# Reordered work at the first layer's beginning and at the layer change of a fused attention and two-layer expert kernel

## The chip, the cores and the metric

One core of a Trainium2 chip runs the whole program. The metric is device time in microseconds, lower is better. The engines are TensorE (PE, with its weight loads as PEld), VectorE (DVE), ScalarE (ACT), GpSimd (POOL) and SyncE (SP), which issues the DMAs.

## The reference

A decayed linear attention over 2 batches of 8 heads and 768 steps gives 1536 tokens of 512 features. They go through a gated layer of 1536 hidden features, and that through four experts of 1024.

```python
state = gamma * state + einsum('bhd,bhe->bhde', k[:, :, t], v[:, :, t])
y[:, :, t] = scale * einsum('bhd,bhde->bhe', q[:, :, t], state)
...
xn = x / rms * rms_g
h = silu(xn @ w_gate) * (xn @ w_val)
x = h @ w_out
...
for e in range(4):
    out += p[:, e:e + 1] * (maximum(x @ w1[e], 0) @ w2[e])
```

All in float32. `silu(g)` is `g / (1 + exp(-g))`, and `p` are the domain probabilities divided by their sum.

## The kernel before

**The arithmetic.** A float32 matmul is made of three: each operand is split into a high part (rounded, made by a copy) and a low part (operand minus high part), and `three` (L616) adds high by high, low by high and high by low in PSUM. On top of this every block product is a 2 by 2 block matrix product made with seven products instead of eight (M1 to M7, `PRODUCTS` for the up projections, `DOWNS` for the first layer's down projection). Its operands are the blocks A11, A12, A22 and four sums S1 to S4 of blocks for the tokens, and B11, B12, B21, B22 and T1 to T4 for the weights. Each of the seven operands of a side needs its own high and low part.

**The stages.** Twelve attention steps (`for n in range(NSTEP)` on each engine) fill `x_all`, and each three of them are normalised as they end. Then the tokens of the first layer come in two halves, `j` = 0 and 1 (the texts call their operand sets k = 0 and 1; k = 2 and 3 are the second layer's), and the hidden features in chunks `c` of 128. An up unit `q` is one chunk by one half: seven products of two k-tiles with three matmuls each, into three PSUM banks, 0 to 2 for even q and 3 to 5 for odd ones. The first units are (c, j) = (0,0), (1,0), (0,1), (1,1), (2,0), (3,0), (2,1), and so on: 24 units (`Q1`) in the first layer. Two units of one half form a pair `r`; its hidden blocks are summed and split too (`hidden_sum`, `hidden_hi`, `hidden_lo`, in four groups: A11; S2 and S3; A22 and A12; S1 and S4), and give 14 down steps (`down1`, L661), which alternate between banks 6 and 7. Step n waits for `posted` to reach n - 1, so a bank must have been taken out before it is written again. The pair's down steps are placed between the products of later units: pair 0's all in unit 3, two after each product (`LATE`), pair 1's in units 4 and 5 (`FIRST`, `SECOND`). The last pairs of the first layer and the second layer use `tile1` and `tile2` in place of the seven products. The second layer's units are 24 and on.

**Who does what.** ScalarE makes the high parts (`part_hi`, `hidden_hi`), copies products that are used twice out of PSUM (`copy_up`: M1, M6, M7 of each unit; M6, M7 and M4 wait for these copies, since they write the same bank), and applies silu. VectorE adds (`c11`, `c22_sum`, `c12`), multiplies (`hidden`), sums tokens and hidden blocks, makes low parts and takes the down steps out of PSUM (`post1`, `post3`, `post2`). GpSimd prepares all weights: four sums (`sum_w`), the high part in one instruction (`split_w_hi`), seven low parts (`split_w_lo`), and some low parts of the tokens, with S3 and once S4 as sums. M3 waits for `c22_ready`.

**What sets the order.** Each engine runs one queue in program order, written out by hand in the stretches that the change touches, with semaphores between engines. GpSimd's stands at L500 to L535: for k = 0 A22 then S3; then four of chunk 1's weights; for k = 1 A11, A12, sum S3, A22, S3, sum S4, S4; the low parts of the down weights (`split_wd_lo(0, 1)`, which first waits for VectorE's one); hidden groups 2 and 3 of pair 0; then the weights of chunk 2, 3, the down weights 1, chunk 4. SyncE's `load_w(c)` (L301) waits until chunk c - 1 has been split, as there is one raw buffer `w_raw` (places 0 to 3 the T sums, 4 to 7 the B blocks). `split_w_hi(c)` waits for the last product of the unit that last read the same of the two buffers. TensorE's order is that of `unit` (L705) with the calls from L726 on; M1 of units 1, 2 and 3 comes two products early, after M7 of the unit before, and the order is the same in both kernels.

## Time and profile before

| | |
|---|---|
| time, median of 3 runs | 842.86 us (842.85 to 845.74) |
| the profiled execution, time | 842.8 us |
| its span, first to last instruction | 841.0 us |
| TensorE busy | 824.5 us, 98% |
| VectorE, ScalarE, GpSimd busy | 549.2, 251.2, 467.7 us |
| TensorE clock granted | 0.999 of full |

Times in rows are microseconds from the span's start. A busy share is an average: this kernel has an attention stage until about 54, the first layer until about 340, overlapping with the second from there to the end. In a timeline, a group's length is from its first start to its last end, and the bracket tells how long the engine had been idle and what released it. Where an instruction waits for several semaphores, the one that came last by the profile is named.

### The profile page before, as it was taken

Reading aid. Unit: us, or ns where it says so; the run is one execution under the profiler, and the core shown is the slowest. Engines: PE = TensorE matmul, PEld = TensorE weight load, DVE = VectorE, ACT = ScalarE, POOL = GpSimd, SP = SyncE. Lnnn points to the kernel's source line nnn. Section 1 sums busy time; section 2 is a strip of 40 time slices with the busy share of each in tenths; the row PEclk is TensorE's granted clock in tenths of the full one; section 3 lists DMA queues with packets and bytes.
Section 4 is the critical chain, followed back from the end, with each engine's and each line's share of the span. In section 5 each row is a group of like instructions: output and inputs, shape, how many; then the busy total and the mean of one; then the engine's idle time right before and its main releaser. Section 6 shows DMA issues by size and latency. Waiting matters only on the chain.

```text
span 841.0 us, 13007 instructions
## 1 busy us (share of the span) xinstructions
PE 824.5 (98%) x4786; PEld 761.2 (91%) x4786; DVE 549.2 (65%) x878; ACT 251.2 (30%) x483; POOL 467.7 (56%) x506
## 2 busy tenths in 40 slices
PE   8998999999999999999999999999999999999998
PEld 8878889999999999789989889899898898898997
DVE  4798978888888868764545545545545545545545
ACT  3586223333333334322222222212212222222221
POOL 3899987968787849932736326326325425425100
PEclk9999999999999999999999999999999999999999
DMA  9801020001010010101100110110110110110003
GB/s 351 315 33 51 1 72 29 26 28 50 26 51 26 26 51 26 51 2 50 52 20 30 51 35 16 51 45 7 50 51 1 51 51 1 51 51 1 25 13 139
DMA packets 12877, 43.17 MB, mean 51 GB/s; under 512 B 1424, under 2 KB 1808, under 8 KB 12816
## 3 DMA queue, kind: packets, MB, share of 16 engines
q1 hardware_dynamic: 12528, 41.69, 14.0%
q8 instruction: 40, 0.66, 0.3%
q10 hardware_dynamic: 288, 0.65, 0.2%
q14 instruction: 21, 0.17, 0.1%
HBM read 39.19 MB, written 3.15 MB: 50 GB/s over the span
## 4 chain that ended last, share of the span: by engine, by line
PE 82%; POOL 9%; DVE 4%; DMA 2%; issue 2%; SPq 1%; ACT 0%; DVEq 0%; POOLq 0%
PE bank L620 27%; PE bank L618 27%; PE bank L619 27%; POOL x_lo L290 3%; POOL w_lo L399 2%; DMA ring<-qkv 2%; POOL w_raw L370 2%; POOL x_sum L286 1%; POOL wd_lo L440 1%; DVE x_sum L286 1%; POOL w_hi L392 1%; POOL h_lo L459 0%; DMA w_raw<-wu 0%; PE bank L547 0%; DVE x_lo L290 0%
## 5 line engine op out<-in xcount | busy, mean ns | idle before, releaser
L618 PE MATMUL bank<-x_hi,w_hi 128*128 128x384 f32 x784 | 264.2, 337 | 7.3 <-POOL w_lo L399 2.9
L620 PE MATMUL bank<-x_lo,w_hi 128*128 128x384 f32 x784 | 262.9, 335 | 0.0
L619 PE MATMUL bank<-x_hi,w_lo 128*128 128x384 f32 x784 | 262.8, 335 | 0.0
L1212 DVE SCALAR_TENSOR_TENSOR out_acc<-bank,p_norm,out_acc 128x512 f32<-128x512 f32 (+1 forms) x181 | 135.1, 747 | 127.2 <-PE bank L620 126.9
L618 PEld LDWEIGHTS bank<-x_hi,w_hi 128*128 128x128 f32 x784 | 147.2, 188 | 15.6 <-issue 6.7
L399 POOL TENSOR_TENSOR w_lo<-w_raw,w_hi 128x256 fp32r<-128x256 f32 x196 | 151.2, 806 | 3.0 <-ACT w_hi L761 0.8
L619 PEld LDWEIGHTS bank<-x_hi,w_lo 128*128 128x128 f32 x784 | 147.2, 188 | 5.5
L620 PE MATMUL bank<-wd_lo,h_hi 128*128 128x512 f32 (+1 forms) x386 | 152.0, 394 | 0.0
L619 PE MATMUL bank<-wd_hi,h_lo 128*128 128x512 f32 (+1 forms) x386 | 151.6, 393 | 0.0
L618 PE MATMUL bank<-wd_hi,h_hi 128*128 128x512 f32 (+1 forms) x386 | 150.0, 389 | 1.4 <-DVE out_acc L1208 1.2
L620 PEld LDWEIGHTS bank<-x_lo,w_hi 128*128 128x128 f32 x784 | 147.1, 188 | 0.0
L446 POOL TENSOR_SCALAR wd_hi<-wd_raw 128x1024 fp32r<-128x1024 f32 x17 | 18.6, 1096 | 209.2 <-DMA wd_raw<-wd 209.2
L794 ACT ACTIVATE u<-bank 128x384 f32<-128x384 f32 x112 | 55.1, 492 | 192.8 <-PE bank L620 192.7
L370 POOL TENSOR_TENSOR w_raw<-w_raw 128x256 f32<-128x256 f32 x112 | 91.2, 836 | 19.9 <-DMA w_raw<-wu 17.7
L820 ACT ACTIVATE h_hi<-bank 128x384 fp32r<-128x384 f32 x96 | 47.3, 492 | 137.9 <-PE bank L620 64.8
L620 PEld LDWEIGHTS bank<-wd_lo,h_hi 128*128 128x128 f32 x386 | 72.4, 188 | 15.2
L618 PEld LDWEIGHTS bank<-wd_hi,h_hi 128*128 128x128 f32 x386 | 72.5, 188 | 14.6 <-issue 2.8
L392 POOL TENSOR_SCALAR w_hi<-w_raw 128x1792 fp32r<-128x1792 f32 x26 | 46.3, 1780 | 69.6 <-PE bank L620 68.9
L619 PEld LDWEIGHTS bank<-wd_hi,h_lo 128*128 128x128 f32 x386 | 72.4, 188 | 11.9
L1158 DVE SCALAR_TENSOR_TENSOR h_lo<-bank,h_hi 128x384 fp32r<-128x384 f32 x96 | 53.2, 554 | 43.0 <-ACT h_hi L820 43.0
L1187 DVE TENSOR_TENSOR x_all<-bank,x_all 128x384 f32<-128x384 f32 x124 | 63.8, 549 | 2.8 <-PE bank L620 2.7
L794 ACT ACTIVATE m<-bank 128x384 f32<-128x384 f32 x56 | 27.5, 491 | 126.0 <-PE bank L620 126.0
(86 smaller groups left out, 994.2 us busy)
## 6 DMA issues: line engine op xcount, KB each, us to landing
w_raw<-wu SPq DMA_DIRECT2D x28, 512.0 KB, 4.4
ring<-qkv SPq DMA_DIRECT2D x23, 512.0 KB, 9.1
wd_raw<-wd SPq DMA_DIRECT2D x22, 512.0 KB, 3.6
out<-out_acc SPq DMA_DIRECT2D x11, 256.0 KB, 2.0
ring<-qkv ACTq DMA_DIRECT2D x1, 512.0 KB, 7.4
y_first<-t_y_decay SPq DMA_DIRECT2D x1, 256.0 KB, 8.0
out<-out_acc SPq DMA_DIRECT2D x2, 128.0 KB, 1.8
small_sb<-small ACTq DMA_DIRECT2D x1, 126.0 KB, 5.2
```

The costliest lines, as they stand in the source:

```text
L290: return engine.tensor_tensor(x_lo[j][:, XS[name], kt, :], operand(k, name)[:, kt, :], x_hi[j][:, XS[name], kt, :].bitcast(F32), ALU.subtract)
L370: return nc.gpsimd.tensor_tensor(w_raw[:, WS[to], :, :], w_raw[:, WS[a], :, :], w_raw[:, WS[b], :, :], ALU.subtract).then_inc(w_sums, 1)
L392: nc.gpsimd.tensor_scalar(w_hi[c % 2][:, :, :, :], w_raw[:, 0:7, :, :], 1.0, 1.0, ALU.mult, ALU.mult).then_inc(w_hi_ready, 1)
L399: nc.gpsimd.tensor_tensor(w_lo[c % 2][:, WS[ws], :, :], w_raw[:, WS[ws], :, :], w_hi[c % 2][:, WS[ws], :, :].bitcast(F32), ALU.subtract).t ...
L618: pe.matmul(dst, s_hi, m_hi, start=first, stop=False, skip_group_check=True)
L619: pe.matmul(dst, s_lo, m_hi, start=False, stop=False, skip_group_check=True)
L620: return pe.matmul(dst, s_hi, m_lo, start=False, stop=last, skip_group_check=True)
L794: nc.scalar.activation(tile[:, s, :], bank[3 * s][:, 0:TB], ACT.Copy).then_inc(u_copied, 1)
L820: nc.scalar.activation(h2_hi[q % 2][:, v, a, :], src, ACT.Relu).then_inc(hi_ready, 1)
L1158: nc.vector.scalar_tensor_tensor(out=h2_lo[q % 2][:, v, a, :], in0=src, scalar=0.0, in1=h2_hi[q % 2][:, v, a, :].bitcast(F32), op0=ALU.max ...
L1187: nc.vector.tensor_tensor(to, new, to, ALU.add).then_inc(posted, 1)
L1212: nc.vector.scalar_tensor_tensor(out=to, in0=new, scalar=p, in1=to, op0=ALU.mult, op1=ALU.add).then_inc(posted, 1)
```

## The change

- SyncE: the weights of chunk 3 are loaded into a buffer of their own, `w3_raw`, over memory that the squares used, after the last norm and after load 2 has landed. Load 4 then waits for chunk 2's split and load 3's landing, not for chunk 3's split.
- GpSimd: chunk 3's B blocks are read from `w3_raw`, and its high part takes two instructions. S3 comes before A22 for k = 0. `sum_4(1)`, `hidden_lo(0, 2)` and `hidden_lo(0, 3)` and, for k = 2, A22's low part go to VectorE.
- ScalarE: a new `post1` copies steps 0 to 7 of pairs 0 and 1 from banks 6 and 7 to `x_all`; the order of units 2 to 4 is written out; S2 before S3 for k = 1; at the layer change S3 of k = 2 before `hidden_hi3`, and M1 of unit 26 is copied before S4 of k = 3.
- VectorE: `post1` keeps only the additions for these pairs; two waits for down steps are added, in `hidden` and `hidden_sum`, which were implied by its posts before; the order from unit 1 to unit 3 and at the layer change is new.

```diff
@@ -147,6 +147,8 @@
...
+        w3_raw = at("w3_raw", [P, 4, 2, P], F32, LAST)
@@ -299,8 +301,15 @@
...
             def load_w(c):
+                if c == 3:
+                    sp.wait_ge(norm_done, 4)
+                    sp.wait_ge(w_in, 16 * c)
+                    sp.dma_start(w3_raw[:, :, :, :], wu[c]).then_inc(w_in, 16)
+                    return
                 if c >= 1:
-                    sp.wait_ge(w_ready, NP * c)
+                    sp.wait_ge(w_ready, NP * (c - 1 if c == 4 else c))
+                    if c == 4:
+                        sp.wait_ge(w_in, 16 * c)
                 sp.dma_start(w_raw[:, 4:8, :, :], wu[c]).then_inc(w_in, 16)
@@ -366,20 +375,27 @@
...
-            def w_op(to, a, b):
-                return nc.gpsimd.tensor_tensor(w_raw[:, WS[to], :, :], w_raw[:, WS[a], :, :], w_raw[:, WS[b], :, :],
-                                               ALU.subtract).then_inc(w_sums, 1)
+            def w_block(c, name):
...
+                if c == 3 and name[0] == "B":
+                    return w3_raw[:, WS[name] - 4, :, :]
+                return w_raw[:, WS[name], :, :]
...
+            def w_op(c, to, a, b):
+                return nc.gpsimd.tensor_tensor(w_block(c, to), w_block(c, a), w_block(c, b), ALU.subtract).then_inc(w_sums, 1)
...
                 pool.wait_ge(w_in, 16 * (c + 1))
-                w_op("T1", "B12", "B11")
-                w_op("T3", "B22", "B12")
+                if c == 3:
+                    pool.wait_ge(w_ready, NP * c)
+                w_op(c, "T1", "B12", "B11")
+                w_op(c, "T3", "B22", "B12")
...
                 pool.wait_ge(w_sums, 4 * c + 1)
-                w_op("T2", "B22", "T1")
+                w_op(c, "T2", "B22", "T1")
                 pool.wait_ge(w_sums, 4 * c + 3)
-                w_op("T4", "B21", "T2")
+                w_op(c, "T4", "B21", "T2")
@@ -389,14 +405,19 @@
...
                     pool.wait_ge(up_done, up_count(last_unit(c - 2), "M3"))
-                nc.gpsimd.tensor_scalar(w_hi[c % 2][:, :, :, :], w_raw[:, 0:7, :, :], 1.0, 1.0,
-                                        ALU.mult, ALU.mult).then_inc(w_hi_ready, 1)
+                if c == 3:
+                    nc.gpsimd.tensor_scalar(w_hi[c % 2][:, 0:4, :, :], w_raw[:, 0:4, :, :], 1.0, 1.0, ALU.mult, ALU.mult)
+                    nc.gpsimd.tensor_scalar(w_hi[c % 2][:, 4:7, :, :], w3_raw[:, 0:3, :, :], 1.0, 1.0,
+                                            ALU.mult, ALU.mult).then_inc(w_hi_ready, 1)
+                else:
+                    nc.gpsimd.tensor_scalar(w_hi[c % 2][:, :, :, :], w_raw[:, 0:7, :, :], 1.0, 1.0,
+                                            ALU.mult, ALU.mult).then_inc(w_hi_ready, 1)
...
                 for _, _, _, ws, _ in PRODUCTS[first:last]:
-                    nc.gpsimd.tensor_tensor(w_lo[c % 2][:, WS[ws], :, :], w_raw[:, WS[ws], :, :],
+                    nc.gpsimd.tensor_tensor(w_lo[c % 2][:, WS[ws], :, :], w_block(c, ws),
                                             w_hi[c % 2][:, WS[ws], :, :].bitcast(F32),
@@ -451,14 +472,6 @@
...
-            def hidden_lo(r, g):
...
-                pool.wait_ge(hid_hi_ready[g], r + 1)
-                pool.wait_ge(hid_sums, 4 * r + 4)
-                for i in range(GROUPS[g].start, GROUPS[g].stop):
-                    lo = nc.gpsimd.tensor_tensor(h1_lo[:, i, :], h1_raw[:, i, :], h1_hi[:, i, :].bitcast(F32), ALU.subtract)
-                lo.then_inc(hid_split[g], 1)
@@ -468,11 +481,6 @@
...
-            def sum_4(k):
-                pool.wait_ge(x_ready["S2"], k + 1)
-                token_sum(nc.gpsimd, k, "S4", slice(0, 1))
-                token_sum(nc.gpsimd, k, "S4", slice(1, 2)).then_inc(sum_ready["S4"], 1)
@@ -500,19 +508,16 @@
...
                     split_w_lo(1, 0, 3)
+            part_lo(0, "S3")
             part_lo(0, "A22")
-            part_lo(0, "S3")
             split_w_lo(1, 3, NP)
...
             part_lo(1, "S3")
-            sum_4(1)
             part_lo(1, "S4")
             split_wd_lo(0, 1)
-            hidden_lo(0, 2)
-            hidden_lo(0, 3)
             for p in range(1, D1):
@@ -525,7 +530,6 @@
...
             part_lo(2, "S3")
-            part_lo(2, "A22")
             split_w(F1 + 1)
@@ -811,6 +815,16 @@
...
+            def post1(r, first, last):
...
+                for i in range(first, last):
+                    n, s = first_part(r) + i, i % 2
+                    _, _, _, _, (half, a) = DOWNS[i // 2]
+                    act.wait_ge(down_done, n + 1)
+                    if r and i == 0:
+                        act.wait_ge(posted, n)
+                    nc.scalar.activation(x_all[r][:, 2 * half + s, a, :], bank[6 + s][:, 0:TB], ACT.Copy).then_inc(posted, 1)
@@ -857,7 +871,8 @@
...
                 s = q % 2
-                copy_up(q, "M1", m1)
+                if q > Q1 + 2:
+                    copy_up(q, "M1", m1)
                 copy_up(q, "M6", u2)
@@ -938,23 +953,45 @@
...
             part_hi(1, "S1")
+            part_hi(1, "S2")
             part_hi(1, "S3")
-            part_hi(1, "S2")
             copy_up(2, "M1", m1)
...
             part_hi(1, "S4")
+            copy_up(2, "M7", u3)
             hidden_hi(0, 0)
-            copy_up(2, "M7", u3)
             hidden_hi(0, 1)
             copy_up(3, "M1", m1)
+            hidden_hi(0, 2)
+            post1(0, 0, 2)
             silu(2, 0)
             silu(2, 1)
-            hidden_hi(0, 2)
             hidden_hi(0, 3)
-            unit1(3)
-            for q in range(4, QP):
+            post1(0, 2, 4)
+            copy_up(3, "M6", u2)
+            post1(0, 4, 6)
+            post1(0, 6, 8)
+            silu(3, 0)
+            copy_up(3, "M7", u3)
+            hidden_hi(1, 0)
+            silu(3, 1)
+            copy_up(4, "M1", m1)
+            hidden_hi(1, 1)
+            copy_up(4, "M6", u2)
+            hidden_hi(1, 2)
+            post1(1, 0, 2)
+            silu(4, 0)
+            copy_up(4, "M7", u3)
+            post1(1, 2, 4)
+            hidden_hi(1, 3)
+            silu(4, 1)
+            post1(1, 4, 6)
+            copy_up(5, "M1", m1)
+            post1(1, 6, 8)
+            unit1(5)
+            for q in range(6, QP):
                 unit1(q)
@@ -969,8 +1006,8 @@
...
             copy_up(Q1, "M1", m1)
+            part_hi(2, "S3")
             hidden_hi3(q, 1)
-            part_hi(2, "S3")
             hidden_hi3(q, 0)
@@ -1001,9 +1038,10 @@
...
             relu_hi(q, 0, 1, bank[3 * (q % 2)][:, 0:TB])
-            part_hi(3, "S4")
             act.wait_ge(c12_ready, q + 1)
             relu_hi(q, 1, 0, bank[3 * (q % 2) + 1][:, 0:TB])
+            copy_up(q + 1, "M1", m1)
+            part_hi(3, "S4")
             for q in range(Q1 + 2, NQ):
@@ -1105,6 +1143,8 @@
...
                     dve.wait_ge(c12_ready, q + 1)
+                    if v == 0 and 0 < q < QP:
+                        dve.wait_ge(down_done, first_part(q // 2 - 1) + 2)
                     x, y = bank[3 * s + 1][:, 0:TB], gate[:, s, :]
@@ -1116,6 +1156,8 @@
...
                 dve.wait_ge(hid_ready, 4 * r + blocks)
+                if to == "S3" and r:
+                    dve.wait_ge(down_done, first_part(r - 1) + 6)
                 if sums:
@@ -1176,15 +1218,12 @@
...
                     n, s = first_part(r) + i, i % 2
-                    name, _, _, _, (half, a) = DOWNS[i // 2]
+                    _, _, _, _, (half, a) = DOWNS[i // 2]
                     d = 2 * half + s
...
                     to, new = x_all[j][:, d, a, :], bank[6 + s][:, 0:TB]
-                    if r < J and name not in ("M2", "M5", "M3"):
-                        nc.vector.tensor_copy(to, new).then_inc(posted, 1)
-                    else:
-                        dve.wait_ge(posted, n - 1)
-                        nc.vector.tensor_tensor(to, new, to, ALU.add).then_inc(posted, 1)
+                    dve.wait_ge(posted, n if r < J and i == 8 else n - 1)
+                    nc.vector.tensor_tensor(to, new, to, ALU.add).then_inc(posted, 1)
@@ -1217,20 +1256,24 @@
...
                 c11(q)
-                post1(r, 0, 2)
+                if r >= J:
+                    post1(r, 0, 2)
                 hidden_sum(r, "S1")
                 c22_sum(q)
-                post1(r, 2, 4)
+                if r >= J:
+                    post1(r, 2, 4)
                 hidden_lo(r, 2)
                 hidden(q, 1)
-                post1(r, 4, 6)
+                if r >= J:
+                    post1(r, 4, 6)
                 c12(q)
...
                 r = q // 2 - 1
-                post1(r, 6, 8)
+                if r >= J:
+                    post1(r, 6, 8)
                 hidden_lo(r, 3)
@@ -1306,29 +1349,28 @@
...
             part_lo(1, "S1")
+            part_lo(1, "S2")
             c11(1)
-            part_lo(1, "S2")
+            sum_of(1, "S4")
             hidden(1, 1)
...
             hidden_sum(0, "S3")
+            c22_sum(2)
             split_wd_lo(0)
+            hidden_lo(0, 0)
+            hidden_sum(0, "S2")
             c11(2)
-            hidden_sum(0, "S2")
-            c22_sum(2)
-            hidden_lo(0, 0)
             hidden_sum(0, "S4")
+            hidden_lo(0, 1)
             hidden_sum(0, "S1")
-            hidden_lo(0, 1)
-            post1(0, 0, 2)
             hidden(2, 1)
             c12(2)
+            hidden_lo(0, 2)
             hidden(2, 0)
-            post1(0, 2, 4)
-            post1(0, 4, 6)
+            hidden_lo(0, 3)
             hidden_sum(1, "S3")
             c11(3)
-            post1(0, 6, 8)
             c22_sum(3)
@@ -1386,8 +1428,8 @@
...
             post3(RP, 6, 7)
+            c22_sum(q)
             part_lo(2, "S1")
-            c22_sum(q)
             post3(RP, 7, 8)
@@ -1401,8 +1443,9 @@
...
             post3(RP + 1, 0, 1)
+            part_lo(2, "A22")
+            part_lo(2, "S4")
             c22_sum(q)
-            part_lo(2, "S4")
             lo11(q)
@@ -1419,20 +1462,20 @@
...
             post2(q - 1, 0)
-            part_lo(3, "S1")
             post2(q - 1, 1)
             lo11(q)
+            c22_sum(q)
             sum_of(3, "S3")
-            c22_sum(q)
+            post2(q - 1, 2)
             lo22(q)
-            post2(q - 1, 2)
+            part_lo(3, "S1")
+            post2(q - 1, 3)
+            lo21(q)
             part_lo(3, "S2")
-            post2(q - 1, 3)
-            sum_of(3, "S4")
-            lo21(q)
             c12(q)
...
             post2(q - 1, 4)
+            sum_of(3, "S4")
             part_lo(3, "S3")
...
             part_lo(3, "S4")

```

## Rows read from the trace of the kernel before

**Rows 1.** The page: busy time by engine, and one costly group: busy, mean ns.

```profile
PE 824.5 (98%) x4786; PEld 761.2 (91%) x4786; DVE 549.2 (65%) x878; ACT 251.2 (30%) x483; POOL 467.7 (56%) x506
...
L794 ACT ACTIVATE u<-bank 128x384 f32<-128x384 f32 x112 | 55.1, 492 | 192.8 <-PE bank L620 192.7
```

**Rows 2.** Windows: stretch, its length, each engine's busy us (instructions), clock, DMA.

```profile
50.00:100.00 50.00, 44.91 (x276) 40.25 (x272) 45.44 (x65) 28.25 (x52) 48.80 (x46) 1.00 0.07 22
...
100.00:120.00 20.00, 17.92 (x101) 17.61 (x102) 16.23 (x27) 6.05 (x11) 16.17 (x20) 1.00 0.12 36
...
120.00:140.00 20.00, 20.00 (x118) 19.99 (x117) 17.12 (x31) 6.61 (x12) 16.91 (x19) 1.00 0.12 45
```

**Rows 3.** Timeline, TensorE 60 to 115, its stalls: start, length, line, [idle before <-releaser].

```profile
62.49 0.41 PE L618 MATMUL bank<-x_hi,w_hi 128*128 128x384 f32 x1 [0.51 <-POOL x_lo L290]
...
76.75 0.41 PE L618 MATMUL bank<-x_hi,w_hi 128*128 128x384 f32 x1 [1.35 <-DVE x_lo L290]
...
82.66 0.41 PE L618 MATMUL bank<-x_hi,w_hi 128*128 128x384 f32 x1 [1.51 <-issue]
...
88.30 0.41 PE L618 MATMUL bank<-h_hi,wd_hi 128*128 128x384 f32 x1 [0.96 <-POOL wd_lo L440]
...
100.05 0.41 PE L618 MATMUL bank<-h_hi,wd_hi 128*128 128x384 f32 x1 [0.58 <-DVE x_all L1187]
...
113.82 0.45 PE L618 MATMUL bank<-x_hi,w_hi 128*128 128x384 f32 x1 [2.02 <-POOL w_lo L399]
```

**Rows 4.** Timeline, GpSimd 58 to 108, instructions of one line merged (x count).

```profile
58.46 1.95 POOL L290 TENSOR_TENSOR x_lo<-x_all,x_hi 128x384 fp32r<-128x384 f32 x2
...
75.74 2.71 POOL L290 TENSOR_TENSOR x_lo<-x_sum,x_hi 128x384 fp32r<-128x384 f32 x2
...
78.42 2.48 POOL L286 TENSOR_TENSOR x_sum<-x_all,x_sum 128x384 f32<-128x384 f32 x2
...
83.78 5.88 POOL L440 TENSOR_TENSOR wd_lo<-wd_raw,wd_hi 128x256 fp32r<-128x256 f32 x6
...
89.62 3.93 POOL L459 TENSOR_TENSOR h_lo<-h_raw,h_hi 128x384 fp32r<-128x384 f32 x4
...
107.64 3.56 POOL L370 TENSOR_TENSOR w_raw<-w_raw 128x256 f32<-128x256 f32 x4 [3.58 <-DMA w_raw<-wu]
```

**Rows 5.** Timeline, VectorE 74 to 108, operations with both inputs in SBUF.

```profile
74.78 1.82 DVE L290 TENSOR_TENSOR x_lo<-x_sum,x_hi 128x768 fp32r<-128x768 f32 x1 [0.36 <-ACT x_hi L789]
...
83.14 1.10 DVE L1127 TENSOR_TENSOR h_lo<-h_raw,h_hi 128x384 fp32r<-128x384 f32 x1
...
86.19 1.49 DVE L1127 TENSOR_TENSOR h_lo<-h_raw,h_hi 128x768 fp32r<-128x768 f32 x1
...
107.21 0.55 DVE L1121 TENSOR_TENSOR h_raw<-h_a,h_raw 128x384 f32<-128x384 f32 x1
```

**Rows 6.** Timeline, ScalarE 80 to 83.

```profile
80.93 0.84 ACT L789 ACTIVATE x_hi<-x_sum 128x768 fp32r<-128x768 f32 x1 [2.37 <-POOL x_sum L286]
...
82.09 0.47 ACT L794 ACTIVATE u<-bank 128x384 f32<-128x384 f32 x1
```

**Rows 7.** Timeline, TensorE 320 to 360, its stalls at the layer change.

```profile
323.56 0.41 PE L618 MATMUL bank<-x_hi,w_hi 128*128 128x384 f32 x1 [0.31 <-DVE c L1085]
...
330.48 0.41 PE L618 MATMUL bank<-x_hi,w_hi 128*128 128x384 f32 x1 [0.41 <-POOL x_lo L290]
...
338.92 0.44 PE L618 MATMUL bank<-x_hi,w_hi 128*128 128x384 f32 x1 [0.92 <-POOL w_lo L399]
...
351.93 0.47 PE L618 MATMUL bank<-wd_hi,h_hi 128*128 128x512 f32 x1 [0.21 <-DVE out_acc L1208]
...
358.74 0.47 PE L618 MATMUL bank<-wd_hi,h_hi 128*128 128x512 f32 x1 [0.46 <-DVE out_acc L1208]
```

**Rows 8.** Timeline, GpSimd and VectorE 330 to 362.

```profile
330.30 1.97 POOL L290 TENSOR_TENSOR x_lo<-x_all,x_hi 128x384 fp32r<-128x384 f32 x2
...
361.44 0.74 DVE L1208 TENSOR_SCALAR out_acc<-bank,p_norm 128x512 f32<-128x512 f32 x1
```

## The prediction, made before the changed kernel ran

> **What bounds the kernel now.** I read the page's busy shares first: TensorE is busy 98% of the span, so only what it idles can be won [rows 1]. The windows then say where: 44.91 of 50 us are busy between 50 and 100, 17.92 of 20 between 100 and 120, and all 20 between 120 and 140 [rows 2]. In that last window 118 matmuls start, two of them across its borders, so one comes every 0.172 us: a product of an up unit (six matmuls) takes 1.04 us, a down step (three) 0.52. The timeline of TensorE last. Idle time in brackets is counted from the modelled end of the matmul before (0.33 after its start, where the next would have started after 0.17), and the first matmul after it is 0.08 longer; so a stall costs its idle time plus about 0.25. In the first layer's beginning six stalls are shown [rows 3], 6.93 idle, with 6 x 0.25 some 8.4 us. At the layer change seven follow each other, five of which are shown [rows 7]; with the two between them, about 4.8 us. Everything that this change can win is in these 13 us, because the remaining matmuls are the same ones at the same clock.
>
> I name a product M3(2) for M3 of up unit 2, and a pair's low part by its operand, as S4 of k=1.
>
> **The change, in the first layer.**
> 1. M7(0) waited for GpSimd's low part of S3, which came after A22's. A22 takes from 58.46 to 60.4 and S3 the next 1.97 [rows 4]. With S3 first, it is there at 60.4; TensorE wants it at 61.8. The stall of 0.51 goes, 0.7 to 0.8 us. A22, now at 62.35, is wanted only two products later, 63.9.
> 2. M6(2) waited for VectorE's low part of S2 [rows 3]. ScalarE now makes S2's high part before S3's, and VectorE the low one before c11. With VectorE's stream 0.8 earlier, S1's low part ends at about 73.05 and S2's, 1.3 to 1.8 long, at 74.3 to 74.9. So M6(2) starts near 74.6 instead of 76.75, and M7(2) would at 76.7. But M7(2) reads S3 of k=1, which GpSimd ends at 78.45 [rows 4]; GpSimd has no idle time from 58.46 on, and only the order of its work changed up to there. So M7(2) starts at 78.5 against 78.8 (76.75 plus two products): of the 2.2 us won here about 0.4 stays, and stall 2 becomes a stall at M7(2).
> 3. M4(2) waited for ScalarE's copy of M7(2) at 82.09, which stood behind the high part of S4 at 80.93, released by GpSimd's sum S4 (78.42, 2.48 long) [rows 4, 6]. VectorE now makes that sum after c11(1), 75.1 to 76.7, and ScalarE's high part is over by 77.6. The copy then waits only for M7(2) itself: 79.7 to 80.2. M4(2) starts at 80.6 against 82.66: 2.0 us won so far. S4's low part on GpSimd ends at 80.4, wanted by M3(2) at 81.65.
> 4. VectorE's own chain comes next. c22 of unit 2 now stands ahead of the first low part of the down weights, and waits for that same copy: 80.2 to 80.7. Then the weights' low part 0.45 (GpSimd is idle, waiting for just this), the low part of hidden A11 1.0, sum S2 1.05, c11 0.5, sum S4 1.05, the low part of group 1 1.45: these are the durations under GpSimd's load [rows 5], against 0.55 where GpSimd rests. They end at 86.2. Down steps 0 and 1 run at 82.7; M5(3) ends at 84.8; steps 2 and 3 want group 1, so a stall of 1.4 stands where 0.96 stood. They start at 86.2 against 88.30: 2.1 us won. ScalarE's two copies of down 0 and 1 end at 86.3 at worst and are not later.
> 5. From there the posts are ScalarE's, 0.49 us each [rows 1], in place of VectorE's of about 0.5. ScalarE is 30% busy, but each copy stands in its queue between waits. Working the queue through, down 4 waits some 0.2 us for post 2 behind the high part of group 3, M4(3) 0.3 for the copy of M7(3) behind a silu, down 12 0.35 for VectorE's post 10. Three small stalls, with restarts about 1.4 us of loss, take the place of the 0.58 at 100.05 and a short one before it.
> 6. M1(5) waited for GpSimd's weights of chunk 3 [rows 3]. GpSimd loses sum S4 (2.45 us) and the hidden low parts (3.93), and the 3.58 us wait for the DMA [rows 4], since chunk 3 now lands in a place of its own from about 69 on. It gains a wait of 0.8 for VectorE's step 4 and one more issue, 0.1. Its down-weight low parts (5.88) run from 81.2 to 87.05; chunk 2's work, which began at 93.5, begins there, and chunk 3's at about 97.5 instead of 107.64. Its first low part stood 6.2 us behind that: 103.7. TensorE wants M1(5) at 109.2. The stall of 2.02 goes entirely, with 5 us of cover.
> Sum: M1(5) at 109.2 against 113.82, so **4.6 us**. On SyncE's queue load 3 now waits for the last norm and load 2's landing, long past; load 4 waits for chunk 2, 97.5, and is early. The two waits added to VectorE's hidden steps are for down steps over 2 us old: nothing.
>
> A VectorE subtraction over 384 columns, both inputs in SBUF, takes 0.55 while GpSimd waits for a DMA and 1.1 while it works [rows 5]. In the Trainium skill, the page "SBUF — State Buffer", section "Who interferes with whom", calls the shared port pair an exclusive lock, so that a VectorE instruction with two SBUF inputs and a GpSimd one that reads SBUF follow each other. By that rule, which the rows bear out, moving the two hidden low parts does not shorten the sum of both engines' work. It gives the second rival its mechanism.
>
> **The layer change.** M3(23) gets its c22 before S1's low part: 0.5 us, of which M2(24) gives back 0.3, as its A12 on GpSimd ends at 327.4 as before. M7(24) waits for S3 behind it: 330.2 against 330.48, won 0.3. A22's low part leaves GpSimd (330.30, 1.97), so the next weights are ready 2 us earlier and the stall of 0.92 at 338.92 is over: M1(25) at 337.6, won 1.3. VectorE has room for A22 at 330.7 to 332.1; M4(24) wants it at 333.4. In unit 25, c22 and the second-layer posts stand before the low parts of S1 and S2; four stalls from 351.93 to 358.74 go, 1.41 idle and four restarts, 2.4 us [rows 7]. But the post of tile 4 (361.44 before [rows 8]) now stands behind both low parts, c12 and lo12, by my sum 358.4 to 359.1, where the first tile of unit 26 wants it at 358.4: with its restart 0.7 us given back. Sum 1.3 + 2.4 - 0.7 = **3.0 us**, bounds 0.5 and 4.5.
>
> Together 7.6 us. The profiled execution took 842.8 for a span of 841.0, and the median of the three runs is 842.86; so span 833.4, and 835.2 in time.
>
> **The rivals.** (a) The forecast, 835.2; own range 832 to 838. (b) The port: VectorE's chain of step 4 has nine SBUF steps before down 12, at 1.1 us under load but up to 1.7 where two GpSimd instructions pass first (S2's low part of 768 columns took 1.82 [rows 5]). Half a microsecond more on six of them is 3 us; the first layer wins 1.6, all together 838.2. For it: VectorE sets three of my four remaining stalls. Against: TensorE's own down steps give slack at most of them. (c) The layer change only moves its stalls to the posts behind the low parts, and wins nothing: 842.8 - 4.6 = 838.2. (d) Both: GpSimd was never the bound, the end moves by under 4 us, 839 to 842. (e) My small new stalls don't occur and the port favours VectorE: 1.4 and 0.7 us more and up to 1 at M7(2), 832. (f) Slower: ScalarE's copies come late. Sixteen posts of pairs 0 and 1 stand between high parts and silus that wait for VectorE, and VectorE's new waits for down steps close the ring. If each of the eight pairs of copies missed its slot by one product and one down pair (2.1 us), 16.8 us are lost against 7.6 won: 852. It decides from 1.5 us a pair on. Against it: by the sum the copies are later than wanted only once, by 0.2.
>
> **How the numbers follow.** Chances: (a) 0.56, (b) 0.13, (c) 0.12, (d) 0.08, (e) 0.07, (f) 0.04. The time is that of (a). The range takes (a) with its bounds, (b), (c), and most of (e): 831.5 to 840. Half a per cent, 4.2 us, is about what a measurement of this kernel tells from no change: faster by more than that holds (a), (e), and most of (b) and (c), 0.79; within it (d) and the rest, 0.17; slower (f), 0.04.
>
> **What would show it.** Right: no idle time at M7(0); one stall before M7(2) at about 78.5, released by GpSimd's low part; GpSimd at its chunk 3 sums before 100 with no DMA wait; M1(5) near 109 without a stall; M1(26), which follows the pair of tiles at 358.74 before, 8.4 us earlier (4.6 + 3.8), and one stall at unit 26's first tile. Wrong: M1(5) later than 111.5 (step 4 or 5), down steps released by ScalarE's copies with a microsecond each (f), or a new stall after 115, where none is now.

## The result, and the profile after

The changed kernel takes 834.87 us (median of 4 runs) against 843.72 for the kernel before beside it, a ratio of 0.9893 with a 95% interval of 0.9877 to 0.991. Measured once more, it was 835.02 against 844.23, 0.9891 (0.9872 to 0.991). The profiled execution took 835.23 us, its span 833.4, which is 7.6 us less than before. The forecast was 835.2 us and a span of 833.4. The medians differ by 8.9 us, which is more than the spans do; the last section shows why (many executions of the kernel before lost some of TensorE's clock).

That the sum is right says little of its terms, so the trace is read in the same order as before. First the page's busy times: ScalarE has 7 us more, the sixteen copies, and VectorE and GpSimd 4 to 5 less each. TensorE is busy 3.2 us less for the same 4786 matmuls, and idle 4.4 less. Of the 3.2 us, 1.2 lie before 60.4, where both kernels take equally long (57.27 and 56.05 busy), so they come from how the ends of matmuls are modelled. The other 2.2 lie where stalls went, 1.1 between 60.4 and M1(5) (46.25 and 45.12) and 1.1 at the layer change (37.15 and 36.10), and are time won: the first matmul behind a stall also takes longer, 0.41 in place of 0.33.

```profile
PE 821.3 (99%) x4786; PEld 760.2 (91%) x4786; DVE 544.8 (65%) x866; ACT 258.3 (31%) x499; POOL 462.9 (56%) x499
```

The windows of TensorE alone (stretch, length, busy us, instructions, granted clock, DMA share, GB/s) find its idle time in the first of these stretches and none in the second, where [rows 3] had the two stalls of 0.58 and 2.02.

```profile
60.00:92.00 32.00, 28.87 (x160) 1.00 0.16 50
92.00:116.00 24.00, 24.00 (x139) 1.00 0.07 23
```

The timeline of TensorE after answers to [rows 3, 7]. Three stalls with a named releaser are left in the first layer's beginning and three at the layer change. The first, at M6(2), ends with ScalarE's copy of M1(2) and not with VectorE's low part of S2, for which the forecast had it wait. M1(5) stands at 108.67 (113.82 before), and M1(26) at 352.52.

```profile
75.27 0.41 PE L622 MATMUL bank<-x_hi,w_hi 128*128 128x384 f32 x1 [0.73 <-ACT m L798]
79.66 0.41 PE L622 MATMUL bank<-x_hi,w_hi 128*128 128x384 f32 x1 [2.06 <-POOL x_lo L292]
86.48 0.41 PE L622 MATMUL bank<-h_hi,wd_hi 128*128 128x384 f32 x1 [0.34 <-DVE h_lo L1169]
...
108.67 0.40 PE L622 MATMUL bank<-x_hi,w_hi 128*128 128x384 f32 x1
...
322.94 0.41 PE L622 MATMUL bank<-x_hi,w_hi 128*128 128x384 f32 x1 [0.69 <-POOL x_lo L292]
325.60 0.41 PE L622 MATMUL bank<-x_hi,w_hi 128*128 128x384 f32 x1 [0.30 <-POOL x_lo L292]
...
351.05 0.47 PE L622 MATMUL bank<-wd_hi,h_hi 128*128 128x512 f32 x1 [0.55 <-DVE out_acc L1247]
...
352.52 0.34 PE L622 MATMUL bank<-x_hi,w_hi 128*128 128x384 f32 x1
```

GpSimd after answers to [rows 4]. The DMA wait of 3.58 us is gone: load 3 goes out at 69.77 (L307). But chunk 3's sums start at 101.00, 6.6 us earlier than before, not 10. Between 70 and 109 several groups take longer than their like did before: the second of the rows below, A22's low part, is 3.41 long, where S3's in [rows 4] took 2.71.

```profile
70.49 3.43 POOL L288 TENSOR_TENSOR x_sum<-x_all 128x384 f32<-128x384 f32 x2
73.88 3.41 POOL L292 TENSOR_TENSOR x_lo<-x_all,x_hi 128x384 fp32r<-128x384 f32 x2
77.25 4.20 POOL L292 TENSOR_TENSOR x_lo<-x_sum,x_hi 128x384 fp32r<-128x384 f32 x4
82.60 6.09 POOL L461 TENSOR_TENSOR wd_lo<-wd_raw,wd_hi 128x256 fp32r<-128x256 f32 x6 [1.15 <-DVE wd_lo L1189]
88.65 4.70 POOL L385 TENSOR_TENSOR w_raw<-w_raw 128x256 f32<-128x256 f32 x4
...
101.00 4.11 POOL L385 TENSOR_TENSOR w_raw<-w_raw 128x256 f32<-128x256 f32 x4
105.20 1.06 POOL L409 TENSOR_SCALAR w_hi<-w_raw 128x1024 fp32r<-128x1024 f32 x1
106.21 1.54 POOL L410 TENSOR_SCALAR w_hi<-w_raw 128x768 fp32r<-128x768 f32 x1
```

VectorE's chain of step 4 answers to [rows 5]. It starts 1.4 us later than forecast and has an idle 2.91 us ahead of it.

```profile
81.57 0.56 DVE L1123 TENSOR_TENSOR c<-bank,u 128x384 f32<-128x384 f32 x1 [2.91 <-ACT u L798]
82.04 0.41 DVE L1189 TENSOR_TENSOR wd_lo<-wd_raw,wd_hi 128x256 fp32r<-128x256 f32 x1
82.37 0.55 DVE L1169 TENSOR_TENSOR h_lo<-h_raw,h_hi 128x384 fp32r<-128x384 f32 x1
82.84 1.10 DVE L1163 TENSOR_TENSOR h_raw<-h_raw 128x384 f32<-128x384 f32 x1
83.86 0.55 DVE L1116 TENSOR_TENSOR bank<-bank,m 128x384 f32<-128x384 f32 x1
84.33 0.63 DVE L1163 TENSOR_TENSOR h_raw<-h_raw 128x384 f32<-128x384 f32 x1
85.06 1.32 DVE L1169 TENSOR_TENSOR h_lo<-h_raw,h_hi 128x768 fp32r<-128x768 f32 x1
```

ScalarE answers to [rows 6]: S3's high part at 73.95 now holds the copy of M1(2) at 74.70, and the copies of the down steps (L826) follow each other without trouble.

```profile
73.95 0.85 ACT L793 ACTIVATE x_hi<-x_sum 128x768 fp32r<-128x768 f32 x1 [1.60 <-POOL x_sum L288]
74.70 0.47 ACT L798 ACTIVATE m<-bank 128x384 f32<-128x384 f32 x1
...
85.83 0.86 ACT L826 ACTIVATE x_all<-bank 128x384 f32<-128x384 f32 x2
```

Three questions follow. Do the two places add up as said? What holds M1(5) now, with how much cover, given that GpSimd came 3.5 us later than I had it and nothing was lost? And what are the moves between engines worth, one by one?

A note on reading positions. The first layer begins up to 0.7 us earlier or later from run to run (its first product after the norm starts between 59.82 and 60.50), so where two kernels are compared inside the first layer, places are counted from M6(2), where the order ahead of it is the same. Spans of one kernel differ too: those of the changed kernel, nine executions, lie between 832.4 and 834.1. The kernels with one edit taken back were not timed beside the changed kernel; their medians are compared with its 834.87, so a difference of some tenths shows nothing.

### The profile page after: what moved, and what is told of

The parts are those of the page before. It is cut to its first block, busy times and chain, and to the rows that moved or that the text cites. A ratio compares the mean times of both kernels' runs of the same rounds, so it can differ in the third digit from the quotient of the medians.

```text
span 833.4 us, 13017 instructions
## 1 busy us (share of the span) xinstructions
PE 821.3 (99%) x4786; PEld 760.2 (91%) x4786; DVE 544.8 (65%) x866; ACT 258.3 (31%) x499; POOL 462.9 (56%) x499
## 4 chain that ended last, share of the span: by engine, by line
PE 88%; POOL 5%; DVE 3%; DMA 1%; issue 1%; ACT 0%; SPq 0%; DVEq 0%
PE bank L622 29%; PE bank L624 29%; PE bank L623 29%; POOL x_lo L292 3%; DMA ring<-qkv 1%; POOL w_lo L420 1%; POOL x_sum L288 1%; PE bank L551 1%; DVE h_lo L1169 0%; PE bank L571 0%; PE bank L564 0%; POOL ring L369 0%; DVE wd_raw L1175 0%; POOL squares L376 0%; POOL w_raw L385 0%
## 5 line engine op out<-in xcount | busy, mean ns | idle before, releaser
L385 POOL TENSOR_TENSOR w_raw<-w_raw 128x256 f32<-128x256 f32 x112 | 93.3, 854 | 16.5 <-DMA w_raw<-wu 14.2
L413 POOL TENSOR_SCALAR w_hi<-w_raw 128x1792 fp32r<-128x1792 f32 x25 | 44.6, 1784 | 68.9 <-PE bank L624 68.3
```

The costliest lines, as they stand in the source:

```text
L385: return nc.gpsimd.tensor_tensor(w_block(c, to), w_block(c, a), w_block(c, b), ALU.subtract).then_inc(w_sums, 1)
L413: nc.gpsimd.tensor_scalar(w_hi[c % 2][:, :, :, :], w_raw[:, 0:7, :, :], 1.0, 1.0, ALU.mult, ALU.mult).then_inc(w_hi_ready, 1)
```

## The experiments

| kernel | median us (beside before) | ratio, 95% interval | span |
|---|---|---|---|
| first layer only | 837.38 (842.42) | 0.9936 (0.9917 to 0.9956) | 835.6 |
| shared w_raw | 836.49 (842.42) | 0.9927 (0.9907 to 0.9947) | 834.2 |
| S3 before A22, k = 1 | 834.30 (842.42) | 0.9899 (0.9877 to 0.9922) | 832.6 |
| posts on VectorE | 838.97 (842.42) | 0.9957 (0.9944 to 0.997) | 837.8 |
| hidden low parts on GpSimd | 836.79 (843.67) | 0.9917 (0.9895 to 0.9939) | 834.7 |
| sum S4 on GpSimd | 836.16 (843.67) | 0.9911 (0.9889 to 0.9933) | 834.8 |
| low parts off the port | 833.25, one run | | 831.5 |
| four orders | 833.45 (843.67) | 0.988 (0.986 to 0.9899) | 831.6 |
| layer change only | 841.14 (844.23) | 0.9966 (0.9951 to 0.9981) | 839.3 |
| own buffer only | 840.71 (844.23) | 0.9962 (0.9947 to 0.9978) | 838.9 |
| changed kernel again | 835.02 (844.23) | 0.9891 (0.9872 to 0.991) | 833.2 |
| four orders again | 832.96 (844.23) | 0.987 (0.9852 to 0.9889) | 831.2 |

### The two places apart

The first layer's edits alone leave out these and the other hunks at the layer change:

```diff
-            c22_sum(q)
             part_lo(2, "S1")
+            c22_sum(q)
             post3(RP, 7, 8)
```

> The change without its edits at the layer change. Theory (the two places add up, each worth what the traces of before and after show): M1 of unit 5 starts at 108.7 as in the changed kernel, and the first product of unit 26 at 355.1, 5.1 us before its place in the kernel before (360.21) and 2.6 us behind the changed kernel (352.52); span 836.0. Rival (the layer change's edits win only because the first layer ended earlier, or win nothing of their own): the same stalls in a new phase, unit 26 within 0.5 us of 352.5, span 833.4 to 833.9.

Its mirror is the kernel before with only those hunks.

> The kernel before with the edits at the layer change alone, the mirror of the run with the first layer alone. Theory (the two places are independent): the first layer's stalls as before, M1(5) where it was, 37.1 us after M6(2); at the layer change the stalls of the changed kernel; span 841.0 less 2.2 to 2.6, 838.4 to 838.8. Rival (the gain at the change needs GpSimd or VectorE to come in earlier): span 840 to 841.

Of the kernel with the first layer alone, one stall that [rows 7] have too, and M1(26); then M1(5) and M1(26) of the kernel with the layer change alone.

```profile
333.60 0.44 PE L623 MATMUL bank<-x_hi,w_hi 128*128 128x384 f32 x1 [0.93 <-POOL w_lo L420]
...
354.81 0.33 PE L623 MATMUL bank<-x_hi,w_hi 128*128 128x384 f32 x1
```

```profile
114.64 0.44 PE L617 MATMUL bank<-x_hi,w_hi 128*128 128x384 f32 x1 [2.48 <-POOL w_lo L399]
...
358.40 0.33 PE L617 MATMUL bank<-x_hi,w_hi 128*128 128x384 f32 x1
```

In the first, M1(26) is at 354.81, 0.3 from the expected 355.1, with the old stall of 0.93 at the new weights; the end lies 2.2 us behind the changed kernel. In the mirror, M1(5) to M1(26) takes 358.40 - 114.64 = 243.76 us, and in the changed kernel 352.52 - 108.67 = 243.85; before it was 360.21 - 113.82 = 246.39 (the pair of tiles at 358.74 in [rows 7] ends at 360.21). So the layer change is worth 2.5 to 2.6 us wherever the first layer ends, and the places are independent. The mirror's span, 839.3, is 0.5 above its range, and its first layer isn't that of the kernel before: M1(5) came at 114.64, 0.8 later, and 38.8 us after M6(2) where 37.1 was expected. Of its ten executions six had spans of 837.5 to 839.3 and four, at a granted clock of 0.996 to 0.998, of 840.4 to 841.1.

### What holds M1(5)

Chunk 3's own buffer taken away:

```diff
-                if c == 3:
-                    sp.wait_ge(norm_done, 4)
-                    sp.wait_ge(w_in, 16 * c)
-                    sp.dma_start(w3_raw[:, :, :, :], wu[c]).then_inc(w_in, 16)
-                    return
                 if c >= 1:
-                    sp.wait_ge(w_ready, NP * (c - 1 if c == 4 else c))
+                    sp.wait_ge(w_ready, NP * c)
```

> The change without chunk 3's own buffer: load 3 waits again until chunk 2 is split, and the high part is one instruction. Theory (GpSimd's weights of chunk 3 are now just in time, no cover is left): load 3 goes out at 100.9, lands near 104.4, the sums take 3.6 to 4.1, the high part 1.8, the first low part 0.75, so M1 of unit 5 starts at 110.6 to 111.2 instead of 108.7 with a stall of about 2: span 2.0 to 2.5 us longer. Rival (the cover of 5 us of the prediction): the 3.5 us wait is swallowed, M1 of unit 5 at 108.7, span within 0.3 us.

GpSimd, and the stall of TensorE, in this kernel:

```profile
103.73 3.75 POOL L370 TENSOR_TENSOR w_raw<-w_raw 128x256 f32<-128x256 f32 x4 [3.52 <-DMA w_raw<-wu]
```

```profile
110.11 0.44 PE L601 MATMUL bank<-x_hi,w_hi 128*128 128x384 f32 x1 [1.93 <-POOL w_lo L399]
```

M6(2) is at 74.64 here, so M1(5) stands 35.47 after it, against 33.40 in the changed kernel: 2.07 later, inside the theory's 1.9 to 2.5. The prediction's cover of 5 us falls; it was 0.1 (in the changed kernel the first low part, 0.74 long, starts at 107.84 and M1(5) at 108.67). (The span is only 0.8 longer: this run started 0.6 earlier, and a stall of the changed kernel at 290.79, 0.43 beyond the usual spacing, which comes and goes from kernel to kernel, isn't in it. The medians differ by 1.6. So by the span alone the theory's 2.0 to 2.5 is missed.)

The buffer alone, on the kernel before:

> The kernel before with chunk 3's own buffer alone, its high part in two instructions, all orders as before. Theory (the 3.58 us wait for the DMA stood in GpSimd's stream ahead of the stall of M1(5)): chunk 3's sums start at about 104.1, two high parts and the first low part end at 110.9 to 111.3, TensorE wants M1(5) at 111.6: the stall of 2.02 goes whole; M1(5) 34.9 to 35.1 us after M6(2) instead of 37.1, span 838.6 to 839.0. Rival (VectorE's posts and hidden low parts would hold M1(5) anyway, or the longer sums under VectorE's load eat it): a stall of 0.5 to 1.5 stays, span 839.3 to 840.5.

```profile
104.23 4.17 POOL L385 TENSOR_TENSOR w_raw<-w_raw 128x256 f32<-128x256 f32 x4
...
109.50 0.84 POOL L410 TENSOR_SCALAR w_hi<-w_raw 128x768 fp32r<-128x768 f32 x1
110.42 5.83 POOL L420 TENSOR_TENSOR w_lo<-w_raw,w_hi 128x256 fp32r<-128x256 f32 x7
```

```profile
111.79 0.45 PE L639 MATMUL bank<-x_hi,w_hi 128*128 128x384 f32 x1
```

M1(5) at 111.79 instead of 113.82, and the span 2.1 shorter, as the theory has it. The matmul ahead of it started 0.32 before it, 0.15 more than the usual 0.17, so the weights are just in time here too. About two fifths of the first layer's 5.15 us is this one wait. Counted from M6(2) the theory misses, 36.4 us instead of 34.9 to 35.1, because M6(2) came 1.3 earlier in this run and a second stall took that back before M4(2).

The hidden low parts back on GpSimd:

```diff
             split_wd_lo(0, 1)
+            hidden_lo(0, 2)
+            hidden_lo(0, 3)
```

> The changed kernel with the low parts of pair 0's hidden groups 2 and 3 made by GpSimd again, after the down weights, as before. Places are given from M6 of unit 2 on (75.27 in the changed kernel), as the starts of the runs differ by some tenths. Theory (the weights of chunk 3 are ready just when M1 of unit 5 wants them, 33.4 us after M6(2)): 3.9 us more on GpSimd, less 0.5 to 1 for a port that VectorE uses less; M1(5) at 36.3 to 37.3 with a stall of 2.5 to 3.5 released by a low part of the weights; span 2.5 to 3.9 us longer. Rival (the prediction's cover of 5 us): M1(5) at 33.0 to 33.8, span within 0.5 us.

```profile
88.46 4.26 POOL L480 TENSOR_TENSOR h_lo<-h_raw,h_hi 128x384 fp32r<-128x384 f32 x4
92.67 2.97 POOL L385 TENSOR_TENSOR w_raw<-w_raw 128x256 f32<-128x256 f32 x4
```

```profile
110.68 0.45 PE L632 MATMUL bank<-x_hi,w_hi 128*128 128x384 f32 x1 [1.32 <-POOL w_lo L420]
```

Neither side is right. M1(5) stands 110.68 - 75.07 = 35.6 after M6(2), 2.2 later than in the changed kernel, and GpSimd had 4.26 us more to do. The theory expected 36.3 to 37.3, the rival 33.0 to 33.8. The span is 1.3 us longer and the median 1.9, where the theory had 2.5 to 3.9. Half comes back: chunk 2's four sums take 2.97 here and 4.70 in the changed kernel, where VectorE makes its two hidden low parts beside them (88.46 to 90.92). Moving 3.93 us of work off GpSimd frees it of about 2.2.

### The port between VectorE and GpSimd

```diff
-            part_lo(1, "S1")
-            part_lo(1, "S2")
+            for name in ("S1", "S2"):
+                dve.wait_ge(sum_ready["S2"], 2)
+                dve.wait_ge(x_hi_ready[name], 2)
+                for kt in range(2):
+                    lo = nc.vector.tensor_tensor(x_lo[1][:, XS[name], kt, :], operand(1, name)[:, kt, :],
+                                                 bank[7][:, 0:TB], ALU.subtract)
+                lo.then_inc(x_ready[name], 1)
```

> The changed kernel with VectorE's low parts of S1 and S2 for k = 1 replaced by four subtractions over 384 columns whose second input is bank 7 in PSUM instead of the high part in SBUF; it leaves out the right low part of these two operands. Theory (GpSimd stands behind VectorE instructions with two SBUF inputs): GpSimd's sum S3, 3.43 for two instructions in the changed kernel, takes 2.0 to 2.7, and A22's low part, 3.41, takes 2.0 to 2.9; the stall before M7(2), 2.06, falls to 0.3 to 1.3. Rival (GpSimd's instructions are slower there for another reason, such as their operands): 3.2 to 3.5 for both, and the stall stays at 1.9 to 2.1.

```profile
70.06 2.72 POOL L288 TENSOR_TENSOR x_sum<-x_all 128x384 f32<-128x384 f32 x2
72.75 2.74 POOL L292 TENSOR_TENSOR x_lo<-x_all,x_hi 128x384 fp32r<-128x384 f32 x2
```

This kernel leaves out the right low parts of S1 and S2, so only its times are read. Both GpSimd groups fall from 3.43 and 3.41 to 2.72 and 2.74, though nothing of GpSimd was touched: the first lies 0.02 above the theory's 2.0 to 2.7, the second in its range, and both far from the rival's 3.2 to 3.5. Each pair of instructions had lost 0.7 us beside VectorE's operations with both inputs in SBUF. The stall before M7(2) falls from 2.06 to 1.1, inside its range. This is the reason for the 1.2 us by which GpSimd came late at M7(2). By the Trainium skill, page "SBUF — State Buffer", section "Who interferes with whom", a VectorE instruction with two SBUF inputs contends with a GpSimd one that reads SBUF, and one with at most one SBUF input, outside the modes that use both ports, doesn't; this run agrees, 3.43 against 2.72 us.

The sum S4 back on GpSimd:

```diff
             part_lo(1, "S3")
+            sum_4(1)
             part_lo(1, "S4")
```

> The changed kernel with the sum S4 of k = 1 made by GpSimd again, between S3 and S4. Theory: the copy of M7(2) stands again behind S4's high part in ScalarE's queue; S4's sum ends 2.0 to 2.5 us after S3's low part, its high part 0.9 later, so M4 of unit 2 starts 1.3 us later than in the changed kernel, M3 of unit 2 at 9.3 us from M6(2) instead of 7.6, and the end 1.5 to 2.2 us later: span 1.5 to 2.2 us longer. Rival (the later VectorE chain to the hidden low part of group 1 sets the place of down step 2 and swallows it): down step 2 at 11.2 to 11.6 from M6(2) as in the changed kernel (11.2), span within 0.5 us.

```profile
73.22 2.69 POOL L292 TENSOR_TENSOR x_lo<-x_all,x_hi 128x384 fp32r<-128x384 f32 x2
75.86 1.97 POOL L292 TENSOR_TENSOR x_lo<-x_sum,x_hi 128x384 fp32r<-128x384 f32 x2
77.79 2.29 POOL L288 TENSOR_TENSOR x_sum<-x_all,x_sum 128x384 f32<-128x384 f32 x2
```

```profile
83.50:86.90 3.40, 3.40 (x12) 0.53 0.00 0
```

Without VectorE's sum beside it, A22's low part takes 2.69 instead of 3.41, so M7(2) comes at 77.97, 1.0 us earlier by the count from M6(2). The theory overlooked this. (It also means that A22's 0.7 us went to two neighbours together, S2's low part and the sum S4: without either of them it takes 2.7.) M4(2) is at 81.44, only 0.3 later by that count instead of 1.3, and M3(2) at 83.34, 8.7 after M6(2) instead of 7.6. The span is 1.4 longer, 0.1 under the theory's range, and the medians differ by 1.3. The rival is out, as M1(5) comes 2.2 later by that count (110.25). Most of this, though, isn't the stalls' own time: the window (TensorE's columns as above) shows the granted clock at 0.53 from 83.5 to 86.9, the lower of its two levels, 1.2 GHz. Its twelve matmuls came every 0.32 us, which lost about 1.5. The other three executions, at a granted clock of 0.999 and 1.0, have spans of 833.9, 833.9 and 834.8, against 832.4 to 833.5 (median 833.2) of the seven of the changed kernel at these clocks. So without the clock the move of the sum is worth about 0.7 us.

### The posts on ScalarE

```diff
-            post1(0, 0, 2)
             silu(2, 0)
             silu(2, 1)
             hidden_hi(0, 3)
-            post1(0, 2, 4)
```

(on ScalarE, and the six calls after them; VectorE makes the copies at the places of before)

> The changed kernel with the sixteen copies of the down steps of pairs 0 and 1 made by VectorE again, at the places that they had before. Theory (the copies had to leave VectorE because it takes the hidden low parts of groups 2 and 3 now): 16 x 0.47 = 7.5 us more on VectorE between 86 and 112, where it idles about 5; down steps wait for posts and low parts, M1 of unit 5 at 110 to 112, span 1.5 to 3.5 us longer. Rival (the copies cost the same on either engine, since GpSimd sets M1 of unit 5 anyway): M1 of unit 5 within 0.4 us of 108.7, span within 0.4 us.

TensorE's stall at down step 4, and the windows around it (for every engine its busy us and instructions, then the clock):

```profile
90.83 0.41 PE L622 MATMUL bank<-h_hi,wd_hi 128*128 128x384 f32 x1 [1.93 <-DVE x_all L1218]
```

```profile
88.00:92.20 4.20, 2.27 (x14) 1.98 (x13) 3.72 (x8) 1.01 (x2) 4.03 (x6) 1.00 0.00 0
92.20:95.70 3.50, 3.50 (x13) 3.50 (x12) 3.50 (x4) 0.00 (x0) 3.42 (x3) 0.52 0.00 0
95.70:99.00 3.30, 3.30 (x21) 3.29 (x20) 2.68 (x7) 1.48 (x4) 3.30 (x6) 1.00 0.00 0
```

The rival is out: the span is 4.4 us longer and the medians differ by 4.1, more than the theory's 3.5; M1(5) is at 112.56, beyond its 110 to 112. Down step 4 waits 1.93 for VectorE's post 2, VectorE is busy 3.72 of 4.2 us, and ScalarE 1.01. Then, behind the stall, the clock is at its lower level for 3.5 us, 13 matmuls in place of 21, about 1.5 us of the 4.4. All six executions of this kernel had a granted clock of 0.998. Without the clock the theory's range holds. So with the hidden low parts on VectorE the posts had to leave it. In the kernel before, VectorE had the posts and not these low parts, and its down steps waited for posts by 0.21 and 0.58 only; that the two moves are one is argued from this, since no run puts both back in the changed kernel.

### Better orders

With S3 ahead of A22 on GpSimd for k = 1:

```diff
-            part_lo(1, "A22")
             part_lo(1, "S3")
+            part_lo(1, "A22")
```

> The changed kernel with GpSimd making S3's low part ahead of A22's for k = 1 as well; everything else alike. Both theories: the stall of 2.06 before M7 of unit 2 goes, M7 starts near 77.5 instead of 79.66. Theory (GpSimd's stream bounds the first layer's beginning, and only its idle 1.15 us before the down weights can be won): M1 of unit 5 starts at 107.6 to 108.1, now with a stall of its own of 1 us or more released by a low part of the weights; span 0.6 to 1.1 us shorter. Rival (the stall before M7 of unit 2 sets the end): M1 of unit 5 at 106.3 to 106.6, span 2.1 to 2.3 us shorter.

```profile
81.95 0.41 PE L622 MATMUL bank<-x_hi,w_hi 128*128 128x384 f32 x1 [0.82 <-POOL x_lo L292]
85.77 0.41 PE L622 MATMUL bank<-h_hi,wd_hi 128*128 128x384 f32 x1 [0.45 <-DVE h_lo L1169]
```

The stall of 2.06 before M7(2) goes, and the span is 0.8 shorter, not 2.1 to 2.3: the rival is out. But the theory's mechanism is half wrong. M1(5), at 108.28, is later than its 107.6 to 108.1 and has no stall of its own. By the count from M6(2), M7(2) comes 1.95 us earlier than in the changed kernel, M3(2) 0.8, down step 2 0.6 and M1(5) 0.3. What was won is lost at M3(2), which waits for S4's low part, still the same GpSimd stream, at down step 2, which waits for VectorE's low part, and at a late down step (96.73). So the exchange itself is worth 0.3 us; of the span's 0.8, 0.4 is the stall near 290, which this kernel doesn't have, and 0.1 an earlier start. M1(5) was merely one of several places that bound this stretch.

Three more orders with it:

```diff
+            copy_up(2, "M1", m1)
             part_hi(1, "S3")
-            copy_up(2, "M1", m1)
...
+            split_wd_lo(0)
             c22_sum(2)
-            split_wd_lo(0)
...
+            post3(RP, 7, 8)
             part_lo(2, "S1")
-            post3(RP, 7, 8)
```

> The changed kernel with four orders exchanged: GpSimd S3 before A22 for k = 1; ScalarE copies M1(2) before S3's high part; VectorE makes the first low part of the down weights before c22 of unit 2; and at the layer change the post of tile 7 comes before S1's low part. Theory (each of them removes a wait that the traces show, the rest of GpSimd's stream stays): M6(2) 0.6 us earlier, no stall at M7(2), M1(5) 0.6 to 1.0 earlier, M2 of unit 24 another 0.9 earlier; span 831.2 to 832.4, 1.0 to 2.2 us shorter than the changed kernel. Rival (only the exchange of S3 and A22 counts): span 832.4 to 832.9.

```profile
107.62 0.45 PE L622 MATMUL bank<-x_hi,w_hi 128*128 128x384 f32 x1
...
321.15 0.41 PE L622 MATMUL bank<-x_hi,w_hi 128*128 128x384 f32 x1
```

M1(5) comes at 107.62, 1.05 earlier (0.8 of it won, the first layer having begun 0.24 earlier), and has a small stall again, 0.26 beyond the usual spacing. M2(24) is at 321.15 against 322.94, with 0.26 where 0.86 was; but a stall of 0.52 is new behind it, at 322.96. From M1(5) to M1(26) this kernel needs 0.8 us less, 0.4 of them the stall near 290, which it doesn't have. M7(2) still waits, 0.50. The span of 831.6 lies in the theory's range. The last comparison puts both kernels on one chip:

> The changed kernel again, beside the one with four orders exchanged: 8.5 to 9.5 us faster than before by the median, span 833.2 to 833.8.

> The kernel with four orders exchanged again: span 831.4 to 832.0, its median 1.0 to 2.2 us below that of the changed kernel in this call. If it is not below, the gain of its trace is within what two builds differ by.

832.96 against 835.02 us, with spans of 831.2 (0.2 below its range) and 833.2. So this version is 2.1 us faster than the changed kernel.

## Why the prediction was right, step by step

| step | forecast | measured |
|---|---|---|
| M7(0) stall | gone | gone |
| M6(2) | 74.6 | 75.27 |
| M7(2), after GpSimd's S3 | 78.5 | 79.66 |
| M4(2), two products after M7(2) | 80.6 | 81.81 |
| VectorE's chain, c22 to group 1's low part | 6.0 long | 4.8 (81.57 to 86.38) |
| down step 2 | 86.2 | 86.48 |
| small stalls from there to M1(5) | 1.4 | 0.2 |
| chunk 3's sums on GpSimd | 97.5 | 101.0 |
| cover of M1(5) | 5 | 0.1 |
| M1(5) | 109.2, won 4.6 | 108.67, won 5.15 |
| M1(25), won at the layer change | 1.3 | 0.8 (332.95; 338.92 before; less 5.15) |
| M1(25) to M1(26), won | 2.4 | 1.7 (21.29 before, 19.57 after) |
| given back from M1(26) on | 0.7 | 0.1 |
| whole layer change | 3.0 | 2.5 |
| span | 833.4 | 833.4 |

The mechanisms held: which stall goes, which comes in its place (S3 at M7(2)), that GpSimd's stream and VectorE's chain set the first layer's beginning, that ScalarE's posts cost TensorE next to nothing (0.15 us at down step 4), that the layer change keeps one stall at a post. The exact hit is luck, since several sizes were off and cancelled: the first layer gave 0.55 more and the layer change 0.5 less. Of the signs that the prediction named, GpSimd at chunk 3's sums before 100 failed (101.0), M7(2) came 1.2 later than its 78.5, and M1(26) 7.7 us earlier instead of 8.4.

**The cover of step 6 was mis-sized.** I let GpSimd's work keep the durations that it had before and only start earlier. It starts earlier beside a VectorE that now holds more work with two SBUF inputs, so S3's sum and A22's low part took 3.4 each where I had about 2.7, and chunk 2's sums 4.70 where 3.3. That is 3.5 us at chunk 3, and S3's lateness of 1.2 at M7(2) is part of it. Chunk 3's own sums and its two high parts took another 1.4 more (the second high part 1.54, where it took 0.84 in the kernel with the buffer alone): its first low part ended at 108.6, where the sum had 103.7. The text itself stated that the moves don't shorten the sum of both engines' work, put it down as rival (b), and then left it out of the sum. It did no harm because the cover was there to be used up, all but 0.1. The runs without the buffer and with the low parts back on GpSimd lose 2.1 and 2.2 us at M1(5), where a cover of 5 would have lost little or nothing.

**Step 2 had the wrong wait at M6(2).** S2's low part was over at 74.74, as forecast (74.3 to 74.9), but M6(2) stood until 75.27 for ScalarE's copy of M1(2), behind S3's high part. It cost nothing, as M7(2) waited for S3 anyway.

**Step 4 was too slow by 1.2.** I priced each operation of VectorE at its loaded duration. But GpSimd was idle, waiting for the very low part that this chain makes, so the next one (0.55) ran free, and one sum took 0.63. The chain started 1.4 late and ended 0.2 late.

**Step 5 was too dark.** Of three small stalls only that at down step 4 came, 0.15 and its restart. Its sum was also wrong in itself: 0.2, 0.3 and 0.35 with three restarts of 0.25 make 1.6 and not 1.4, and from 86.2 that gives 109.7 for M1(5) and not 109.2 (measured, M1(5) stands 22.2 after down step 2, of which 0.2 is stall).

**The layer change** gave 0.5 less: M2(24) waited 0.69 for A12, since S1's low part (1.64) now runs behind c22, which first waits for ScalarE's copy, and both stand ahead of the post that A12's high part wants (ScalarE began it at 319.25, after 0.66 idle). I had that loss at 0.3. In unit 25 the four stalls went, but another of 0.55, at the last tile before unit 26, I hadn't seen; against it, the stall forecast at unit 26's first tile was 0.12 and not about 0.7. The forecast also said that no stall stood after 115 in the kernel before. One does, 0.24 idle at 295.94, and the changed kernel has its like (0.26 at 290.79), so it didn't count.

Rival (b) describes what happened on GpSimd, not on VectorE. Rival (c) is out by the kernels with one place each, and rival (e) was right on the small stalls, 1.2 us, and wrong at M7(2). Rival (f) is refuted by the copies' rows and by the span. Of the moves, the buffer alone gave 2.0 at M1(5); undoing the posts alone costs 4.1 by the medians, the hidden low parts alone 1.9, and sum S4 1.3. In the profiled executions of the first and the last of these three kernels about 1.5 us is the clock. How the remaining few tenths divide between the orders of ScalarE's high parts and of c11 wasn't tried.

## What to carry to other kernels

When work moves between VectorE and GpSimd, price both streams anew: here VectorE's operations with two SBUF inputs lengthened the GpSimd instructions beside them, so 3.9 us taken off GpSimd freed it of only 2.2. Before calling a wait covered, add up the whole stream that covers it with its durations under the new load, and test the cover by taking one saving away. And look for a wait that stands in a busy engine's stream without any work behind it: a 3.58 us DMA wait, removed by a second buffer, gave 2 us for one extra instruction.
